# The second round's down product by seven quarter products, with weight sums on GpSimd and sums of the activations on VectorE

## The reference

```
xt = x.transpose(0, 2, 1)
h = np.maximum(xt @ w_tok1, 0.0) @ w_tok2
u = x + h.transpose(0, 2, 1)
h2 = np.maximum(u @ w_ch1, 0.0) @ w_ch2      # 768 -> 1536 -> 768
return (u + h2).astype(np.float32)
```

## Time and profile before

| what | value |
|---|---|
| median of 3 runs | 838.54 us (838.15 to 839.6) |
| profiled execution | 837.65 us, its span 835.9 us |
| busy in the span: PE, DVE, ACT, POOL | 827.9, 569.8, 397.6, 115.2 us |
| TensorE's granted clock | 1.00 over the span |
| round 1, down product | 582.9 to 669.4 us |
| round 2, up product | 669.4 to 745.0 us |
| round 2, down product | 745.0 to 831.4 us |
| DMA over the span | 101.7 MB, 122 GB/s |

### The profile page before, as it was taken

One profiled execution on the slowest core, in us unless ns is written; L12 is line 12 of the kernel. 1 busy time (PEld: TensorE's weight loads), 2 busy tenths in 40 slices (PEclk: granted clock), 3 DMA queues, 4 the chain that ended last, 5 costly groups with the idle time before them and its releaser, 6 DMA issues.

```text
span 835.9 us, 12752 instructions
## 1 busy us (share of the span) xinstructions
PE 827.9 (99%) x4976; PEld 716.5 (86%) x4976; DVE 569.8 (68%) x882; ACT 397.6 (48%) x559; POOL 115.2 (14%) x79
## 2 busy tenths in 40 slices
PE   9999999999999999999999999999999999999997
PEld 6545554589999999999999999999999999999997
DVE  5899999989977675864547589778435167771311
ACT  6999999947556554613122234444242144441110
POOL 0253546332000000052422000000000000000000
PEclk9999999999999999999999999999999999999999
DMA  6547665244412221347663452533513165532221
GB/s 173 164 126 198 166 184 141 61 122 103 111 50 61 62 59 29 113 115 216 209 181 106 144 179 73 180 108 114 181 56 123 56 204 156 161 95 57 62 99 67
DMA packets 90380, 101.71 MB, mean 122 GB/s; under 512 B 37680, under 2 KB 88016, under 8 KB 90320
## 3 DMA queue, kind: packets, MB, share of 16 engines
q1 hardware_dynamic: 90096, 100.67, 41.3%
q10 hardware_dynamic: 224, 0.23, 0.1%
HBM read 76.62 MB, written 24.24 MB: 121 GB/s over the span
## 4 chain that ended last, share of the span: by engine, by line
PE 88%; DVE 6%; issue 3%; ACT 1%; POOL 0%; DVEq 0%; POOLq 0%; ACTq 0%
PE psum L1448 26%; PE psum L1447 26%; PE psum L1446 26%; PE psum L1502 4%; PE psum L1458 3%; DVE tile_sums L1007 2%; PE psum L1529 1%; DVE tile_sums L1014 1%; ACT ring L784 1%; DVE kq_lo L994 1%; DVE kq_hi L992 1%; DVE x_t L1020 1%; PE psum L1537 1%; DVE sum_rows L1029 1%; PE psum L1460 1%
## 5 line engine op out<-in xcount | busy, mean ns | idle before, releaser
L1202 DVE TENSOR_TENSOR part_lo<-part_raw,part_hi 128x384 fp32r<-128x384 f32 x132 | 72.5, 553 | 81.4 <-ACT part_hi L879 81.3
L879 ACT ACTIVATE part_hi<-part_raw 128x384 fp32r<-128x384 f32 x132 | 64.5, 516 | 123.8 <-DMA part_raw<-moe_w_ch 114.2
L1448 PE MATMUL psum<-h_hi,part_lo 128*128 128x448 f32 x288 | 104.5, 363 | 0.0
L1447 PE MATMUL psum<-h_lo,part_hi 128*128 128x448 f32 x288 | 104.4, 362 | 0.0
L1446 PE MATMUL psum<-h_hi,part_hi 128*128 128x448 f32 x288 | 103.7, 360 | 0.0
L1448 PE MATMUL psum<-block_hi,part_lo 128*128 128x448 f32 x252 | 91.5, 363 | 0.0
L1447 PE MATMUL psum<-block_lo,part_hi 128*128 128x448 f32 x252 | 91.3, 362 | 0.0
L1446 PE MATMUL psum<-block_hi,part_hi 128*128 128x448 f32 x252 | 90.8, 360 | 0.0
L1502 PE MATMUL psum<-ring,values 128*32 128x448 f32 x768 | 81.4, 542 | 0.4 <-issue 0.3
L784 ACT ACTIVATE ring<-psum,score_scale 128x1344 f32<-128x1344 f32 (+1 forms) x48 | 75.3, 1568 | 9.7 <-PE psum L1460 6.9
L787 ACT ACTIVATE ring<-ring,cap_col 128x1344 f32<-128x1344 f32 (+1 forms) x48 | 77.2, 1608 | 1.6
(11 more groups left out here) (154 smaller groups left out, 2019.0 us busy)
## 6 DMA issues: line engine op xcount, KB each, us to landing
part_raw<-moe_w_ch SPq DMA_DIRECT2D x84, 192.0 KB, 2.3
kq_raw<-kq_t SPq DMA_DIRECT2D x47, 224.0 KB, 3.8
part_raw<-quad_scratch SPq DMA_DIRECT2D x48, 192.0 KB, 2.3
values<-v SPq DMA_DIRECT2D x48, 112.0 KB, 3.4
inverse_rows<-inverse_scratch SPq DMA_DIRECT2D x12, 448.0 KB, 6.2
rows_scratch<-turned SPq DMA_DIRECT2D x112, 48.0 KB, 1.7
x_rows<-rows_scratch SPq DMA_DIRECT2D x28, 192.0 KB, 2.4
block_scratch<-block_turned SPq DMA_DIRECT2D x32, 168.0 KB, 3.3
```

The lines of the kernel that those rows point to most:

```text
L879: act.activation(part_hi[SLOTS[q]][:, :], part_raw[SLOTS[q]][:, :], ACT.Copy).then_inc(part_hi_made, 1)
L1202: dve.tensor_tensor(part_lo[slot][:, :], part_raw[slot][:, :], part_hi[slot][:, :].bitcast(F32), ALU.subtract).then_inc(part_lo_made, 1)
L1447: pe.matmul(out, left[0], right[1], start=False, stop=False)
L1448: return pe.matmul(out, left[1], right[0], start=False, stop=stop)
```

## The change

Round 2's down product is made by seven quarter products too. Quarters are now the even or odd feature tiles (three pairs) by the two column halves, summed over both halves of the hidden units.

- **PE:** `fall_by_seven(m, pair)`: for each of the seven products and each of 3 pairs, 2 parts of 9 matmuls, 18 into one bank. Eight banks go round.
- **Weights:** `w_ch2` comes laid out in quarters. In round 1's down product SP loads 12 half blocks of 4 x 128 x 192 into the place of three blocks that PE has read by then (`load_half_quads`), GpSimd makes four sums of each (`sum_half_quads`), and SP stores them (`store_half_quads`) to `fall_quad_scratch`. From step 7 to 16 of the 24 steps, SP's list has a part load, a store and a load of half blocks each.
- **Activations:** in round 2 `relu_to_hi` makes the relu in place in full precision; `sum_rises` (DVE) makes four sums of a group's quarters in the place in the list where `relu_to_lo` stood; `seven_to_hi` (ACT) and `seven_to_lo` (DVE) split the operands, those of M1 in the last up group, those of every other product while PE makes the product before it.
- **Results:** `add_seven` (DVE) adds every product to the quarters of `x_t`, directly or by the running sum `chain` (1, 1, 2, 3, 1, 2, 1 operations for M1, M2, M6, M7, M4, M5, M3); `copy_first_fall` (ACT) copies M1's products to `chain`. Output goes out by quarters, the last one (M3) by pairs, in three DMAs of 224 KB.
- **Round 1's down product** keeps its arithmetic, with another order: feature half `p`, then half of the hidden groups, then `k`, then feature tile; a part is now one feature tile by three hidden tiles.
- `load_blocks` moves from step 7 to step 20 of that product, `sum_blocks` from steps 4 to 7 to steps 14 to 17, `block_to_lo` from step 9 on to step 17 on.

```diff
-PARTS = C_PAIRS * len(M_ORDER) + FALLS
+RISES = C_PAIRS * len(M_ORDER)
+D_PAIRS = D_TILES // 2
+SEVEN_FALLS = len(M_ORDER) * D_PAIRS * 2
+PARTS = 2 * RISES + FALLS + SEVEN_FALLS
 N_SLOTS = 7
-SLOTS = [3, 0, 1, 2, 3, 0] + [(1, 2, 3, 0, 4, 5, 6)[q % N_SLOTS] for q in range(ROUNDS * PARTS - 6)]
+SLOTS = [3, 0, 1, 2, 3, 0] + [(1, 2, 3, 0, 4, 5, 6)[q % N_SLOTS] for q in range(PARTS - 6)]
 UP_BANKS = ((2, 3, 4, 5, 0, 1), (4, 5, 0, 1, 6, 7))
-FALL_BANKS = (((6, 7, 2, 3, 4, 5), (0, 1, 6, 7, 2, 3)), ((2, 3, 4, 5, 0, 1), (6, 7, 2, 3, 4, 5)))
+FALL_BANKS = ((6, 7, 2, 3, 4, 5), (0, 1, 6, 7, 2, 3))
+SEVEN_BANKS = (2, 3, 4, 5, 0, 1, 6, 7)
+HALF_QUADS, QUAD_BUFFERS = 2 * C_PAIRS, 3
+RELU_OF = {M1: (0, 0), M2: (1, 0), M5: (0, 1), M3: (1, 1)}
+FALL_ADDS = {M1: 1, M2: 1, M6: 2, M7: 3, M4: 1, M5: 2, M3: 1}
...
+def seven_part(m, pair, g_half):
+    return 2 * RISES + FALLS + 2 * D_PAIRS * M_ORDER.index(m) + 2 * pair + g_half
...
+        fall_quads = [place(f"fall_quads{e}", [P, 4, HALF // 2], F32, block_at[T2 + e]) for e in range(QUAD_BUFFERS)]
...
+        chain = [place(f"chain{e}", [P, SEQ], F32, h_at[h_tile(e, 1, 1)]) for e in range(D_PAIRS)]
...
+            def load_seven(m, pair, g_half):
+                q, group = seven_part(m, pair, g_half), 2 * pair + g_half
+                after(sp, part_read, last_use(q))
+                if m in QUADS:
+                    for e in range(QUAD_BUFFERS):
+                        sp.wait_ge(half_quads_stored[e], 16 * HALF_QUADS // QUAD_BUFFERS)
+                    weights = fall_quad_scratch[group, QUADS[m]]
+                else:
+                    weights = w_ch2[group, int(m == M4), int(m != M1)]
+                sp.dma_start(part_raw[SLOTS[q]][:, :], weights).then_inc(part_loaded[SLOTS[q]], 16)
+            def load_half_quads(h):
+                e, columns = h % QUAD_BUFFERS, slice(h % 2 * HALF // 2, (h % 2 + 1) * HALF // 2)
+                after(sp, half_quads_stored[e], 16 * (h // QUAD_BUFFERS))
+                sp.wait_ge(part_read, part_of(0, C_PAIRS - 1, M4) + 1)
+                sp.dma_start(fall_quads[e][:, :, :], w_ch2[h // 2, :, :, :, columns].rearrange("m k p n -> p (m k) n")
...
+            def store_half_quads(h):
+                e, columns = h % QUAD_BUFFERS, slice(h % 2 * HALF // 2, (h % 2 + 1) * HALF // 2)
+                sp.wait_ge(half_quad_steps, 4 * (h + 1))
+                sp.dma_start(fall_quad_scratch[h // 2, :, :, columns].rearrange("q p n -> p q n"),
+                             fall_quads[e][:, :, :]).then_inc(half_quads_stored[e], 16)
...
+            def store_quarter(m, m_half, n):
+                sp.wait_ge(fall_adds_made, fallen(m, D_PAIRS - 1))
+                sp.dma_start(out_t[2 + n].rearrange("(d p) n -> p d n", p=P)[:, m_half:D_TILES:2, :],
+                             x_t[:, 0, m_half:D_TILES:2, n * SEQ:(n + 1) * SEQ]).then_inc(out_stored, 16)
+            def store_last(pair):
+                sp.wait_ge(fall_adds_made, fallen(M3, pair))
+                sp.dma_start(out_t[3, 2 * pair * P:(2 * pair + 1) * P, :], x_t[:, 0, 2 * pair, SEQ:2 * SEQ]
+                             ).then_inc(out_stored, 16)
...
+                if s == 0:
+                    for step in range(FALLS):
+                        load_fall(step // 12, step // 6 % 2, step // 3 % 2, step % 3)
+                        if 5 <= step < 5 + HALF_QUADS + 2:
+                            if step >= 7:
+                                store_half_quads(step - 7)
+                            if step < 5 + HALF_QUADS:
+                                load_half_quads(step - 5)
+                        if step == C_TILES + 8:
+                            load_blocks()
+                            store_fallen(0)
+            for m in M_ORDER:
+                for pair in range(D_PAIRS):
+                    for g_half in range(2):
+                        load_seven(m, pair, g_half)
+                        if (m, pair, g_half) == (M7, 0, 1):
+                            store_quarter(M2, 0, 0)
+                        if (m, pair, g_half) == (M3, 0, 1):
+                            store_quarter(M4, 1, 0)
+            store_quarter(M5, 1, 1)
+            for pair in range(D_PAIRS):
+                store_last(pair)
+            sp.wait_ge(out_stored, 16 * 10)
...
+            def sum_half_quads(h):
+                e = h % QUAD_BUFFERS
+                pool.wait_ge(half_quads_loaded[e], 16 * (h // QUAD_BUFFERS + 1))
+                a11, a12, a21, a22 = [fall_quads[e][:, quad, :] for quad in range(4)]
+                pool.tensor_tensor(a22, a21, a22, ALU.add).then_inc(half_quad_steps, 1)
...
+            for h in range(HALF_QUADS):
+                sum_half_quads(h)
...
+            def seven_to_hi(m, g):
+                act.wait_ge(part_read, part_of(1, C_PAIRS - 1, m) + 1)
+                if m in (M1, M2, M3):
+                    act.wait_ge(relu_made, 4 * g + {M1: 1, M2: 2, M3: 3}[m])
+                else:
+                    act.wait_ge(rise_sums_made, 4 * g + {M7: 1, M6: 2, M4: 3, M5: 4}[m])
+                act.activation(seven_hi[m][g][:, :], seven_raw[m][g][:, :], ACT.Copy).then_inc(seven_hi_made, 1)
+            def copy_first_fall(pair):
+                act.wait_ge(part_read, seven_part(M1, pair, 1) + 1)
+                act.activation(chain[pair][:, :], psum[:, SEVEN_BANKS[pair], 0:SEQ], ACT.Copy
+                               ).then_inc(firsts_copied, 1)
...
+            def sum_rises(g, m):
+                h11, h12, h21, h22 = [h_raw[h_tile(g, m_half, n_half)][:, :] for m_half in range(2)
+                                      for n_half in range(2)]
+                if m == M7:
+                    dve.wait_ge(relu_made, 4 * g + 4)
+                    dve.tensor_tensor(seven_raw[M7][g][:, :], h22, h12, ALU.subtract).then_inc(rise_sums_made, 1)
...
+                else:
+                    dve.tensor_tensor(seven_raw[M5][g][:, :], h12, h11, ALU.subtract).then_inc(rise_sums_made, 1)
+            def seven_to_lo(m, g):
+                dve.wait_ge(seven_hi_made, C_PAIRS * M_ORDER.index(m) + g + 1)
+                dve.tensor_tensor(seven_lo[m][g][:, :], seven_raw[m][g][:, :], seven_hi[m][g][:, :].bitcast(F32),
+                                  ALU.subtract).then_inc(seven_lo_made, 1)
...
+            for step in range(FALLS):
+                part_to_lo(RISES + step + 3)
+                if step == 0:
+                    relu_to_lo(0, C_PAIRS - 1, M3)
+                if step == C_TILES:
+                    add_fallen(0)
+                if 14 <= step < 18:
+                    sum_blocks(1, (T1, T2, T3, T4)[step - 14])
+                if 17 <= step < 17 + N_BLOCKS:
+                    block_to_lo(1, step - 17)
+            part_to_lo(part_of(1, 0, M1) + 3)
+            add_fallen(1)
+            rise(1, 0, M_ORDER[1:])
+            for g in range(1, C_PAIRS):
+                rise(1, g, M_ORDER)
+            for g in range(4, C_PAIRS):
+                seven_to_lo(M1, g)
+            for m in M_ORDER:
+                for step in range(2 * D_PAIRS):
+                    part_to_lo(seven_part(m, 0, 0) + step + 3)
+                    if m == M1 and 1 <= step < 5:
+                        sum_rises(C_PAIRS - 1, (M7, M6, M4, M5)[step - 1])
+                    if m != M3:
+                        seven_to_lo(M_ORDER[M_ORDER.index(m) + 1], step)
+                    if step % 2 == 1:
+                        add_seven(m, step // 2)
...
+            def fall_by_seven(m, pair):
+                r = D_PAIRS * M_ORDER.index(m) + pair
+                if r < 2:
+                    pe.wait_ge(out_made, 11 + r)
+                elif r < 8:
+                    wait_until_read(1, C_PAIRS - 1, M_ORDER[r - 1])
+                elif r - 8 < D_PAIRS:
+                    pe.wait_ge(firsts_copied, r - 8 + 1)
+                else:
+                    pe.wait_ge(fall_adds_made, fallen(M_ORDER[(r - 8) // D_PAIRS], (r - 8) % D_PAIRS))
+                for g_half in range(2):
+                    q = seven_part(m, pair, g_half)
+                    slot = SLOTS[q]
+                    pe.wait_ge(part_lo_made, q + 1)
+                    for third in range(3):
+                        g = 3 * g_half + third
+                        if pair == 0:
+                            pe.wait_ge(seven_lo_made, C_PAIRS * M_ORDER.index(m) + g + 1)
+                        units = slice(third * P, (third + 1) * P)
+                        mm = products(psum[:, SEVEN_BANKS[r % 8], 0:SEQ],
+                                      (part_hi[slot][:, units], part_lo[slot][:, units]),
+                                      (seven_hi[m][g][:, :], seven_lo[m][g][:, :]), g == 0, g == C_PAIRS - 1)
+                    mm.then_inc(part_read, 1)
...
-                for p in range(2):
-                    for c in range(C_TILES):
-                        fall(s, p, c)
+                if s == 0:
+                    for p in range(2):
+                        for g_half in range(2):
```

(33 more changed lines are left out.)

220 lines of the change are left out of this document (142 added, 78 removed).

## The result

| | before | changed |
|---|---|---|
| median | 838.42 us (838.15 to 839.6, 4 runs) | 826.29 us (825.79 to 828.12, 4 runs) |
| ratio | | 0.9857, 95% interval 0.9838 to 0.9875 |
| profiled execution, its span | 837.65, 835.9 us | 828.12, 826.3 us |

What follows compares the result with a forecast made beforehand. TensorE (PE), busy 827.9 of 835.9 us, was taken as the bound. The terms -10.8 + 0.5 - 0.9 = -11.2 us, from the median 838.54, gave 827.3 us, range 825.3 to 831.2.

Steps and rivals of the forecast that it cites:

- PE's list, -10.8: Round 2's down product: 378 matmuls in place of 432, 54 fewer at 0.200 us each, 10.8 us less.
- Round 1's down product in another order, 0: Round 1's down product: same 432 matmuls reordered, results free two at a time, easier for VectorE's adds; 0 us.
- The weight sums, 0: Round 1's down product: GpSimd's sums of 12 half blocks, 0.65 us an operation, 2.6 a block, stay covered; 0 us.
- 12T may be 60.6 us, and T 5.05: Round 1's down product: GpSimd's time T per half block may reach 5.05 us before part 19's load comes late.
- Rival (c): Round 1's down product: SP stands behind GpSimd, part loads late; 843.5 us at 6.4 a block, slower from T = 6.3; chance 0.04.
- The port shared by VectorE and GpSimd: Round 1's down product: VectorE and GpSimd exclude each other; 12 chains cost VectorE 25 us, covered by 49 us idle.
- The blocks' loads, 0: Round 1's down product: round 2's blocks loaded at step 20, awaited until 643.1 us, hold by 2.5 us; 0 us.
- Rival (d): Around 633 us: DMAs (blocks, outputs, half blocks, parts) pile up and give the gain back, about 838 us; chance 0.02.
- VectorE in the last up group, +0.5: Round 2's last up group: PE waits for VectorE's fourth split at the first seven product; 0.5 us more.
- In the seven products, 0: Round 2's down product: VectorE needs 58.6 of 75.6 us, and its lead covers M7's pairs; 0 more on PE.
- Rival (b): Seven products: VectorE late, operations follow by durations (0.55, 0.62) not distances; up to 3.9 in place of 0.5, 830.7 us; chance 0.10.
- The end, -0.9: After the last matmul: last output DMA of 224 KB lands in 2.3 us instead of 3.2; 0.9 us less (0 to 1.5).

## Why the prediction was right, point by point

*PE's list, -10.8:* right. 378 matmuls begin in 76.0 us, 0.200 apart but for the wait; 54 put back cost 10.8 in the trace and 10.5 to 11.4 by timing. The 0.189 us of the Trainium skill ("TensorE: Matmul & The Clock Gate", Back-to-back issue gap), which that page gives for an isolated matmul, doesn't describe this stream: 0.200 is what the rows show before and after. PE's busy time fell by 9.9 us and not by 10.8: the three stretches of the earlier trace rows account for 10.5, and the rest of the kernel, which is unchanged, was 0.6 us busier in this execution.

*Round 1's down product in another order, 0:* right; its stretch is 86.5 us long.

*The weight sums, 0:* right in the result, and 0.65 us an operation is what was measured (31.3 us for 48; 0.60 to 0.80). **Wrong was the bound**, "12T may be 60.6 us, and T 5.05": it looked at part 19, the last thing behind GpSimd, and not at what is due first. At 4.4 us a block PE already waited 5.3 us for the blocks' sums, and at 5.6 us also 8.1 for the adds. Rival (c) therefore has its point of decision lower: 834.0 us at 4.4 a block and 848.5 (one run) at 5.6, so break-even with 838 lies between, where the prediction put it at 6.3. (Its own sum gives 6.0: 5.05 + 11.2 / 12.) The room was there by luck as much as by design, since the bound that was checked wasn't the one that holds.

*The port shared by VectorE and GpSimd:* 0.8 for 0.6 us on GpSimd where the two meet, and without effect on the time, as the run without sums shows. The price on VectorE was put ten times too high: its busy time in that stretch is 39.8 us instead of 37.2, 2.6 us more and not 25. The six splits of the earlier trace rows followed each other without a pause; here VectorE has one split in 3.6 us.

*The blocks' loads, 0:* right for the time, with 0.7 and 1.4 us of room in the two executions instead of 2.5, and none in one execution of a run with an edit elsewhere. Rival (d), DMAs that pile up there and give the gain back, fell: they do pile up (outputs landing in 10.9 us), but the stretch keeps its 86.5 us. The term that was mis-sized is the landing: 11.0 us from SP's first issue to the first sum (10.4 to 12.6 over the runs with the loads at step 20), not 9.8, and SP there 0.7 us later.

*VectorE in the last up group, +0.5:* 0.51. *In the seven products, 0:* no wait of PE but that one. Rival (b), durations instead of distances, fell: the starts lie 0.47 and 0.535 us apart for the new operations as well.

*The end, -0.9:* it was -1.4. From the start of the last matmul to the end of the span are 822.95 to 826.3, 3.35 us, against 4.75 in the earlier trace rows. The landing of 224 KB (all ten output DMAs, against the earlier trace rows) took 1.9 us, not 2.3:

```profile
L737 SPq DMA_DIRECT2D out_t<-x_t x3: 332/333/338, 816.8 to 824.0; - x3
...
DMA to landing us min/median/max: 1.9/4.2/11.1
```

*The sum:* -10.8 + 0.5 - 1.4 = -11.7 us; measured -12.1, within the interval. The missing 0.4 us isn't accounted for, and the timing can't resolve it. The forecast of 827.3 lies 1.0 above the measured median: 0.5 of that is the end, 0.1 the median of before, which is 838.42 with the fourth run, and 0.4 this open rest.

## What to carry to other kernels

On a kernel whose PE never waits, price a matmul by the distance between starts, and trust the product with the number removed; the work of the helpers is free up to a point that has to be worked out. When a queue gets a slow member, list everything behind it with its due time and take the earliest: here it was a block load with about 1 us of room, not the last weight part. A stop of TensorE costs more than its length, so room of 1 us on such a path is worth widening even when the time doesn't show it.

## What I had not expected of the hardware

TensorE's granted clock fell to the lower level after a stop of only 2.6 us, and 8 matmuls then started 0.37 us apart. The length of the slow part doesn't follow that of the stop: it was 8 or 9 matmuls after 5.3, 8.1 and 10.8 us too (GpSimd's chain longer), and 12 after 6.0. Stops of up to 1.2 us (the run with two more operations on VectorE) left it at 1.00. And with the DMA engines at a share of 0.68, an output DMA of 672 KB took 10.9 us to land instead of 4.3, while the 192 KB part loads of the same stretch took 3.5 at the median instead of 2.3.
